# Scaling all score levels of a decay attention straight from the 8-step references, with factors summed on TensorE

## What is computed

```
def _attn_ref(q, k, v, a_re, a_im):
    mag = np.sqrt(a_re * a_re + a_im * a_im)
    scale = np.minimum(mag, 0.999) / (mag + 1e-06)
    a_re_n, a_im_n = (a_re * scale, a_im * scale)
    for t in range(S):
        new_re = ar * S_re - ai * S_im          # ar, ai: step t of a_re_n, a_im_n
        new_im = ar * S_im + ai * S_re
        kv = np.einsum('bhd,bhe->bhde', k[:, :, t], v[:, :, t])
        S_re, S_im = (new_re + kv, new_im)
        y[:, :, t] = np.einsum('bhd,bhde->bhe', q[:, :, t], S_re)

x = relu(x @ w_in) ** 2 @ w_out                 # 384 -> 2048 -> 384
x = (silu(x @ w_gate) * (x @ w_val)) @ w_out2   # 384 -> 1536 -> 384
```

## Time and profile before

| | us |
|---|---|
| median of 3 runs | 1340.24 (1339.74 to 1340.48) |
| the profiled execution, time | 1340.01 |
| its span, first to last instruction | 1338.2 |
| TensorE busy | 1230.1 (92%), 10390 matmul records |
| TensorE weight load busy | 1149.7 (86%) |
| VectorE busy | 773.1 (58%) |
| ScalarE busy | 753.0 (56%) |
| GpSimd busy | 162.8 (12%) |
| mean granted clock of TensorE | 0.957 |
| chain that ended last | TensorE 65%, VectorE 20%, ScalarE 7%, issue 7% |

### The profile page before, as it was taken

The page is one execution under the profiler, slowest core; times in us unless marked ns, Lnnn a source line. Parts: engine busy times, 40 slices in busy tenths (PEclk is TensorE's granted clock), DMA queues, the critical chain, the costliest instruction groups (busy, mean ns, idle before and its releaser), DMA issues.

```text
span 1338.2 us, 26822 instructions
## 1 busy us (share of the span) xinstructions
PE 1230.1 (92%) x10390; PEld 1149.7 (86%) x10390; DVE 773.1 (58%) x1300; ACT 753.0 (56%) x1473; POOL 162.8 (12%) x140
## 2 busy tenths in 40 slices
PE   2566899998999999998999998999999999999998
PEld 2455788888888888888888898999999999999998
DVE  5889788887887878788778840144222222222322
ACT  5665777777877877877778844652222222222221
POOL 1000122122121121121221222300000000000000
PEclk9666899999999999999999997999999999999999
DMA  4321111111111111111211102240101001000000
GB/s 134 115 84 54 37 36 55 55 48 55 50 42 54 54 37 54 54 37 55 59 49 37 42 16 98 72 130 19 36 0 37 18 19 33 3 35 0 18 19 18
DMA packets 42138, 62.53 MB, mean 47 GB/s; under 512 B 3120, under 2 KB 37680, under 8 KB 41648
## 3 DMA queue, kind: packets, MB, share of 16 engines
q1 hardware_dynamic: 42032, 60.98, 14.6%
HBM read 46.81 MB, written 14.16 MB: 46 GB/s over the span
## 4 chain that ended last, share of the span: by engine, by line
PE 65%; DVE 20%; ACT 7%; issue 7%; DVEq 0%; ACTq 0%
PE bank L1340 7%; PE bank L1342 7%; PE bank L1341 7%; PE bank L1363 4%; PE bank L1359 4%; PE bank L1361 4%; PE bank L1248 3%; PE bank L1261 3%; PE bank L1250 3%; PE bank L1249 3%; PE bank L1265 3%; PE bank L1263 3%; PE bank L1181 2%; PE bank L1229 2%; PE bank L1230 2%
## 5 line engine op out<-in xcount | busy, mean ns | idle before, releaser
L433 POOL TENSOR_TENSOR glo<-rg,ghi 128x384 fp32r<-128x384 f32 x128 | 157.6, 1232 | 709.7 <-ACT ghi L598 709.7
L1076 DVE TENSOR_TENSOR prod<-bank,silu 128x384 f32<-128x384 f32 x96 | 53.5, 557 | 285.3 <-PE bank L1342 269.2
L706 ACT ACTIVATE silu<-bank 128x384 f32<-128x384 f32 x84 | 41.4, 493 | 281.1 <-PE bank L1342 281.1
L1248 PE MATMUL bank<-xhi,win_hi 128*128 128x384 f32 x384 | 140.6, 366 | 8.7 <-DVE xlo L964 7.2
L1261 PE MATMUL bank<-ghi,wout_hi 128*128 128x384 f32 x384 | 135.2, 352 | 0.0
L1250 PE MATMUL bank<-xhi,win_lo 128*128 128x384 f32 x384 | 132.6, 345 | 0.0
L1249 PE MATMUL bank<-xlo,win_hi 128*128 128x384 f32 x384 | 132.3, 345 | 0.0
L1265 PE MATMUL bank<-ghi,wout_lo 128*128 128x384 f32 x384 | 129.2, 336 | 0.0
L1263 PE MATMUL bank<-glo,wout_hi 128*128 128x384 f32 x384 | 128.7, 335 | 0.0
L1181 PEld LDWEIGHTS bank<-QT,KT 112*64 112x64 f32 x2304 | 80.5, 149 | 51.2 <-DVE KT L907 20.9
L1181 PE MATMUL bank<-QT,KT 112*64 112x64 f32 x2304 | 90.9, 237 | 33.1 <-DVE KT L907 15.4
(11 more groups left out here) (162 smaller groups left out, 3059.9 us busy)
## 6 DMA issues: line engine op xcount, KB each, us to landing
gates_sb<-in_gates SPq DMA_DIRECT2D x48, 192.0 KB, 2.4
qk_sb<-in_qk SPq DMA_DIRECT2D x24, 384.0 KB, 3.2
v_sb<-in_v SPq DMA_DIRECT2D x24, 192.0 KB, 3.2
xT_scratch<-yT SPq DMA_DIRECT2D x48, 96.0 KB, 2.1
xin<-xT_scratch SPq DMA_DIRECT2D x8, 576.0 KB, 4.1
y1T_scratch<-y1s SPq DMA_DIRECT2D x8, 576.0 KB, 3.5
x<-y1T_scratch SPq DMA_DIRECT2D x8, 576.0 KB, 3.9
out<-o_sb SPq DMA_DIRECT2D x8, 576.0 KB, 2.9
```

The source lines that it names most:

```text
L433: pool.tensor_tensor(glo[:, j % GR, :], rg[:, j % 2, :], ghi[:, j % GR, :].bitcast(F32), ALU.subtract)\
L1248: nc.tensor.matmul(banks[4][:, 0:UT], win_hi[:, k, c], xhi[:, k, :], start=k == 0, stop=False)
```

## The change

- `span_table` replaces the matrix `halves` (16 columns) by 88 columns: for each level and for the start of the chunk, the sum of log decays from an 8-step block's middle to the border that this level needs. One `block_sums` now gives all factors; `block_decays` takes the exponential of 88 rows; D's transposes have 88 columns instead of 32 and go to two banks; `evac_D` copies them in two passes to DT with 11 groups of factors.
- VectorE makes the scaled Q and K of every level directly from QT0, KT0 and DT, with eight passes of 512 elements a partition (`to_borders8` to `to_borders64_K`), alternating between QA, KA and QB, KB; the trees and the in-place chain go. `to_start` scales QT0 in two passes.
- scores8 and scores16 have only 32 columns a matmul, since only the odd blocks of Q are kept.
- Q, K and E tiles are packed: 96 rows (2 x 48) instead of 112 of 128. `state` is split into a matmul of 64 weight columns and one of 32.
- The two masks of `sides` go; ScalarE makes the sign of the real part (`signs`, with a bias of 1e-30), and `phases` is rewritten with it. The gate loads on SyncE wait for it.
- `carry` lies in rows of Dn. Masks are kept for one head and broadcast.
- The order on all engines is written anew. On TensorE: scores, scores8, scores16, slot 0, gate sums, slot 1, block sums, slot 2, scores32, scores64, slots 3 and 4, phase sums, outputs, state, slot 5, all transposes, slots 6 to 10. The order is the same with and without MLP work.

```
--- before.py
+++ after.py
@@ constant_tables
-    halves = s // mid == np.arange(CH // mid)[None, :]
+LEVELS = (8, 16, 32, 64)
+NG = 2 * len(LEVELS) + 3
+ND = NG * 8
+def span_table():
+    s = np.arange(CH)
+    mids = np.arange(0, CH, BLK) + BLK // 2
+    groups = []
+    for L in LEVELS:
+        odd = mids // L % 2 == 1
+        groups.append([(s >= m // L * L) & (s < m) for m in mids[odd]])
+        groups.append([(s >= m) & (s < (m // L + 1) * L) for m in mids[~odd]])
+    to_start = [s < m for m in mids]
+    groups += [to_start[:8], to_start[8:], [s >= 0] + [s < 0] * 7]
+    return np.stack([c for g in groups for c in g], axis=1)
...
@@ scalar
+            def signs(n):
+                act.wait_ge(ev["ucl"], n)
+                act.wait_ge(ev["th0"], n - 1)
+                act.activation(t3[:, :], re_sb, ACT.Sign, bias=tiny[:, :]).then_inc(ev["sign"], 1)
...
+            def evac_D(n):
+                act.wait_ge(ev["sdec"], n - 1)
+                for i in range(2):
+                    act.wait_ge(ev["pDT"], 2 * n - 1 + i)
+                    src = banks[i][0:KR, 0:4 * ND].rearrange("p (h g c) -> p g h c", h=4, c=8)
+                    act.activation(DT[:, :, 4 * i:4 * i + 4, :], src, ACT.Copy).then_inc(ev["DTev"], 1)
...
@@ scalar, unit
                     if nxt:
                         magnitudes(n + 1)
-                    works(ci, (0,), *flags)
+                        high_gates(n + 1)
...
                     if nxt:
                         inverse(n + 1)
-                    if nxt:
-                        high_gates(n + 1)
...
+                    works(ci, (0,), *flags)
                     if nxt:
                         decays(n + 1)
+                    works(ci, (1,), *flags)
                     if ci == 0 and has_head:
                         split_x(u - 1)
-                    works(ci, (3,), *flags)
                     if nxt:
+                        signs(n + 1)
                         block_decays(n + 1)
                         angle(n + 1)
+                    works(ci, (2,), *flags)
                     copy32(n)
-                    works(ci, (4,), *flags)
...
                     copy64(n)
-                    works(ci, (5,), *flags)
+                    works(ci, (3,), *flags)
+                    if nxt:
                         high_theta(n + 1)
...
+                    works(ci, (4,), *flags)
+                    if nxt:
                         sines(n + 1)
                     evac_y(n)
...
-                    works(ci, (7, 8), *flags)
+                    works(ci, (5,), *flags)
...
                     if nxt:
-                        evac_QK(n + 1)
-                    works(ci, (9, 10), *flags)
+                        evac_Q(n + 1)
+                        evac_K(n + 1)
+                        evac_D(n + 1)
+                    works(ci, (6, 7, 8, 9, 10), *flags)
...
@@ vector
-                dve.scalar_tensor_tensor(t2[:, :], t6[:, :], 1.0 / math.pi, t2[:, :], ALU.subtract, ALU.mult)\
+                dve.scalar_tensor_tensor(t2[:, :], t2[:, :], math.pi / 4, t3[:, :], ALU.subtract, ALU.mult)\
...
+            def to_borders8(n):
+                dve.wait_ge(ev["DTev"], 2 * n)
+                dve.wait_ge(ev["QTev"], 2 * n)
+                dve.wait_ge(ev["p32"], n - 1)
+                dve.tensor_tensor(dense(QA, 8), blocks_of(QT0, 8, 1), factors(0, 1), ALU.mult).then_inc(ev["sc8"], 1)
...
@@ tensor
+                for i in range(2):
+                    pe.wait_ge(ev["QTev"], 2 * n - 1 + i)
+                    for h in range(4):
+                        ins = nc.tensor.transpose(banks[i][0:KR, h * ND:(h + 1) * ND], Dn[0:ND, 4 * i + h, :],
+                                                  ident[0:ND, 0:ND])
+                    ins.then_inc(ev["pDT"], 1)
...
                 for h in range(H):
-                    ins = nc.tensor.matmul(banks[2][0:KR, h * D:(h + 1) * D], En[:, h, 0:KR], v_sb[:, ci, h * D:(h + 1) * D],
-                                           start=True, stop=True)
+                    for rows in (slice(0, 64), slice(64, KR)):
+                        ins = nc.tensor.matmul(banks[2][rows, h * D:(h + 1) * D], En[:, h, rows],
+                                               v_sb[:, ci, h * D:(h + 1) * D], start=True, stop=True)
```

More of the change, by code:

```diff
@@ L114, in build @@
         run_sum, last_row, around_mid, suffix = (sums_r[:, i * P:(i + 1) * P] for i in range(4))
[L115 to L128 removed]
+        spans = sums_r[:, 4 * P:4 * P + ND]
+        names = """sq absre sign msq0 msq lnm einv mag tcorr ucl dsum lnrho lnd invd ratio atan th0 theta
             pTheta pF pE pD kk thw absw sinw trig expF expG expE expD qF kG kE Qn Kn En
             lrhi lrlo thhi thlo cyhi cylo r32
[L131 removed]
+            pQT pKT pDT QTev KTev DTev p0 sc8 m0 p8 sc16 m8 p16 sc32 m16 p32 sc64 c32
             p64 scF c64 pY yev pS sdec sadd"""
@@ L312, in load_gates @@
             def load_gates(b, j, n):
[L314 removed]
+                sp.wait_ge(ev["sign"], n - 1)
                 sp.wait_ge(ev["ratio"], n - 1)
@@ L657, in unit @@
                         weight1(i)
-                    works(ci, (6,), *flags)
-                    if nxt and not has_head:
+                    works(ci, (4,), *flags)
+                    if nxt:
                         sines(n + 1)
                     evac_y(n)
-                    if nxt and has_head:
-                        sines(n + 1)
                     if has_next or ci < CPU - 2:
                         squares(n + 2)
-                    works(ci, (7, 8), *flags)
+                    works(ci, (5,), *flags)
                     for i in pieces[2:3]:
@@ L974, in unit @@
                         clear_state(u, c)
-                    to_borders(n)
-                    if nxt and not has_head:
+                    to_borders8(n)
+                    to_borders16(n)
+                    if nxt:
                         capped(n + 1)
@@ L1019, in unit @@
                     if nxt:
+                        wrap(n + 1)
                         rotate(n + 1)
@@ L1137, in block_sums @@
                 pe.wait_ge(ev["expE"], n)
-                sum_hi_lo(banks[1][0:2 * NH8, 0:HD], halves, lnrho_hi[:, :], lnrho_lo[:, :]).then_inc(ev["pD"], 1)
+                sum_hi_lo(banks[1][0:ND, 0:HD], spans, lnrho_hi[:, :], lnrho_lo[:, :]).then_inc(ev["pD"], 1)
             def phase_sums(n, first=False):
@@ L1180, in scores, with pair_scores @@
                         rows = slice(HALF * r, HALF * (r + 1))
-                        ins = nc.tensor.matmul(banks[bank][rows, h * HALF:(h + 1) * HALF], k[:, h, rows],
-                                               q[:, h, rows], start=True, stop=True)
+                        ins = nc.tensor.matmul(banks[2][rows, h * HALF:(h + 1) * HALF], KT0[:, h, rows],
+                                               QT0[:, h, rows], start=True, stop=True)
+                ins.then_inc(ev["p0"], 1)
+            def pair_scores(q, k, L, done):
+                for h in range(H):
+                    for r in range(2):
+                        rows = slice(HALF * r, HALF * (r + 1))
+                        c = PAIRS[L].start + h * 32
+                        ins = nc.tensor.matmul(banks[3][rows, c:c + 32], k[:, h, rows], q[:, h, 32 * r:32 * (r + 1)],
+                                               start=True, stop=True)
```

304 lines of the change are left out of this document (123 added, 181 removed).

## The result

The kernel after takes 1498.94 us (median of 4 runs, 1494.34 to 1501.86) against 1340.36 us before (4 runs, 1339.74 to 1342.95): a ratio of 1.116, with a 95% interval of 1.113 to 1.119. The forecast was 1378 us, with a range up to 1402. The sign was right; the size was not: 159 us lost where 38 were foreseen. The profiled execution after has a span of 1500.1 us.

A forecast was written before the change was run, and what follows sets the result against it. TensorE bounds settled units before; after, the cycle over ScalarE and the block of works does. From 1340 us, +26 for longer chunks gives 1366, and +12 for clock falls gives 1378 us, range 1330 to 1402.

The forecast's parts named there:

- TensorE's savings: TensorE's own work falls 2.0 us a chunk to near 29.6, but the saving does not reach the end.
- the bursts: On TensorE, nine bursts of fp32 matmuls a chunk become four, at 0.2 us each: 1.0 us saved.
- sixteen at 0.70 to 1.08 us give 0.7 to 1.1; I take 1.0: TensorE's state as 16 narrow matmuls takes 1.0 us a chunk in place of 1.77; 0.7 saved.
- The rule of the Trainium skill: Changing tiling mode drains TensorE: up to sixteen drains, 1.6 us, in the state; time 1388 instead of 1378.
- ScalarE's ledger: ScalarE from table load to first Q evacuation, then tails: a unit takes 103.0 us, before 98.5.
- the wait between K's halves: TensorE idle some 1.7 us in chunks 0 and 2, as K's second transposes wait for the first Q copy.
- 7 x 1.7 = +12: The clock falls behind quiet places in 7 of 13 chunks, 1.7 us each: +12 us.
- Rival C: The clock falls in almost every chunk, at both quiet places: 1366 + 44 = 1410 us; chance 0.14.
- The loop gap goes (queued matmuls of the block cover it): TensorE's gap at the loop's turn, 9.0 us in four places before, disappears; not in the 103.0 us unit.
- A: TensorE stays the bound, each settled chunk losing 3.5 us: time near 1271 us; chance 0.12.
- B: The ScalarE cycle holds but round trips overlap better: unit 98 to 100 us, time 1325 to 1350; chance 0.14.
- D: The forecast itself, ScalarE's cycle and the block setting the time: 1350 to 1400 us, likeliest 1378; chance 0.60.

The follow-up runs named there:

- e1: The changed kernel with the state's split undone, one matmul of 96 weight columns a head: 1434.07 us, 1.067 of the kernel before.
- e9: The changed arithmetic with the state whole and the MLP works in the places of the kernel before, on TensorE and ScalarE: 1345.94 us, 1.003.
- e12: e9 with TensorE's loop over the units written out: 1342.4 us, 0.9985 of the kernel before.
- e5: The changed kernel with the split state grouped by width, all matmuls of 64 columns first, then all of 32: 1435.43 us, 1.068.
- e2: The kernel before with only its state split, into 64 and 48 weight columns: 1337.23 us, 0.996.
- e8: e1 with work 6 of chunks 0 and 2 moved ahead of the transposes: 1403.92 us, 1.044.
- e6: The changed kernel with state whole and the works spread in a new order on TensorE and ScalarE, arithmetic unchanged: 1361.45 us, 1.013.
- e3: e1 with eight useless matmuls ahead of each of two TensorE waits (low gates, theta) in chunks 0 and 2: 1412.72 us, 1.051.
- e4: e1 with TensorE's loop over units 2 to 6 written out: 1431.18 us, 1.065.
- e10: e6 with the state's decay and sum moved earlier on VectorE: 1348.63 us, 1.005.

## Why the prediction was right in sign and wrong in size

The loss splits without a large rest. Split of the state 65 us (after to e1), order of the works 88 us (e1 to e9, 1434 to 1346), arithmetic and packing with the orders that e9 keeps about 4 us (e9 to before on its own chip, 0.3%). What the lower clock cost is inside these parts and not a fourth one: the changed kernel had 162 us more of it than the one before (280 against 118), which by the price worked out below is an estimated 50 to 80 us of the loss.

- **TensorE's savings.** Foreseen 2.0 us a chunk, 0.7 of it from the state. By steps of matmuls at the full clock, 200 to 770 us, e12 against before, a chunk: scores of all levels 4.39 against 4.52, state 1.38 against 1.59, gate, block and phase sums 2.27 against 2.39, the MLP items 0.24 less, the transposes of D some 0.1 more. In all 0.6 us where 2.0 were foreseen. Two terms were mis-sized: the level 8 and 16 scores (0.4) saved 0.1, and the bursts (1.0, from one step beside the scores, taken for all) at most the 0.4 of the sums and the MLP items.
- **The state.** The failed step is "sixteen at 0.70 to 1.08 us give 0.7 to 1.1; I take 1.0". It took 3.53 us at the full clock. The bounds were rows of one width repeated; none had two widths in turn. e5 and e2 show that the change between 64 and 32 columns is what costs, and the price was 2.5 us a chunk over the term and 65 us in the sum. The rule of the Trainium skill, TensorEngine Tiling (Array Packing), Key Properties, a drain at each change of tiling mode, was cited in the prediction, priced at up to 1.6 us a chunk and 10 us in the time, and left out of the forecast. The trace of e5 agrees with it (1.72 us for 14 changes); that 48 columns count as the same mode as 64, as e2 suggests, is not shown otherwise. The cover by ScalarE's sines, which I counted as a half, was not there: the state ends behind them (at 431.82; ScalarE then waits 1.57 us, up to 434.13, for the Q transposes behind it).
- **ScalarE's ledger.** Right as a mechanism. The tails came out to 0.3 us, and chunk 1, at the full clock, to 1.5 us in the chain; the 2.5 us of the state above its term are enough for all of that. One piece was mis-sized: the wait between K's halves took 0.76 us in the mean and not 1.7. e8 and e6 confirm that the block counts: moving one item ahead brings 30 us, spreading them 73, the clock's share in it included. Three slips moved nothing: the earlier trace rows give 31.3 us of TensorE work a chunk, so 2.0 less is 29.3 and not 29.6; it is busy 95% of that unit and not 94%; and chunk 0's waits of 3.9 leave 0.1 for a wait said to be 0.3 to 0.9.
- **The clock.** The failed step is "7 x 1.7 = +12". The unit shown has four TensorE waits of 2.0 us or more (2.04, 2.89, 2.74 and 3.83 us). At the first three the clock fell within 0.5 us behind their ends, at the last during the wait. With a fifth fall, behind no such wait, the unit has 37.5 us at the lower clock; the term had one fall of 3.4 us in each of 7 chunks, about one a unit. A fall lengthens ScalarE's waits for MLP banks (5.65 us ahead of 500.06) and so the next wait of TensorE. Before, one unit had one such place. Rival C (falls in almost every chunk) described this, but with 1.7 us a fall it still gave only 1410. What the lower clock cost can be estimated from e1, whose two executions are one program: 1441.53 us at a mean clock of 0.914 and 1426.61 at 0.930, so some 48 us fewer at the lower level (twice the missing share of the time) and 15 us less. By that a microsecond at the lower level costs a third of one. In e3 it costs a half: from one Q transpose to the third after it, stretches with 17.1 us at the lower level take 115.2 to 116.4 us and those with 3.4 take 108.7 to 110.4. For the unit's 37.5 us this is 12 to 19 us, and with 7.5 for three states it covers most or all of the 24.5 us by which the unit exceeds the 103.0 foreseen.
- **The loop's turn.** "The loop gap goes (queued matmuls of the block cover it)" was wrong: 16.7 us in eight places against 9.0 in four. In the changed kernel with its state whole it costs little (e4); with the state split, where it is longest, that was not tried.
- **VectorE and SyncE.** Foreseen 3 us less on VectorE: 22 us busy against 26. No stall came from the gate loads.
- **Rivals.** A (TensorE stays the bound, 1271) has its test in e9: with the works spread TensorE is busy 93% of the time, but 0.6 us a chunk is too little. In e12 a unit has 1.4 us more waits (5.9 against 4.5) and 6.8 us at the lower clock against 3.4, which takes the 2 us a unit back. B (1325 to 1350) and D (1350 to 1400) are out with the measured 1499.

Open: why the clock falls where it does. In e10 a turn of 2.03 us was followed by the full clock; in e12 the lower one was granted for 6.8 us from 519.16, between waits of 0.90 (up to 518.43) and 0.66 us (up to 520.44):

```profile
516.56:520.00 3.44, 3.44 (x99) 3.34 (x100) 1.35 (x3) 2.79 (x5) 0.69 (x1) 1.00 0.02 5
```

```profile
519.16:525.98 6.82, 6.17 (x57) 5.97 (x54) 2.63 (x4) 2.87 (x6) 0.68 (x1) 0.50 0.01 2
```

Ahead of its wait e10 has three MLP items in a row behind the transposes; e12 has transposes with one item between them, and then the scores. The runs do not tell which difference decides; no run changed it alone.

## What to carry to other kernels

Cost an order by following the in-order engine that joins the stages, and then ask what each bare wait of TensorE does to the clock: here the waits of 2 to 4 us in the unit sum to 11.5 us, and the stretches at the lower clock beside them to an estimated 12 to 19. Before a matmul is split, look what the pieces' widths do in turn: 64 and 48 columns went faster than the whole, 64 and 32 much slower; if they clash, group by width or leave it whole. When arithmetic and order change together, run the new arithmetic in the old order first: here e9, beside e1, shows that the arithmetic gave nothing that could be measured and that the order took 88 us.

## What the runs showed that was not expected

- Matmuls of 64 and 32 weight columns in turn cost about 0.12 us a change (3.53 against 1.81 us a chunk at the full clock); 64 and 48 in turn took 1.06 us for sixteen, less than eight of 112 (1.59), and advanced twice as fast a record (30 ns) as 64 after 64 in e5 (58 ns).
- Such a stretch at half the clock took 1.5 times as long (5.39 against 3.53 us); e1's whole state took 1.9 times as long (2.58 against 1.38).
- The turn of TensorE's loop, a wait with no releaser, was 1.3 to 1.5 us in e1, 1.9 to 2.7 before, 1.8 to 2.7 in e10 and 2.4 to 4.4 in e9; where the state had sixteen matmuls it came in two pieces, together 3.6 to 5.1 us. Writing the loop out gave 3 to 12 us.
- The same program on the same chip varied with its mean granted clock: e10 took 1339.34 us at 0.962 and 1352.71 at 0.948.
